# Who makes the low part of g in the early tiles: VectorE alone in the first five, GpSimd from the sixth on

## The reference

```python
w = softmax(weight_gen)                                  # over the 7 taps
conv[b, s, h, :] = sum over k of w[b, s, h, k] * x_pad[b, s + k, h, :]
h = conv @ w_in            # 16384 x 192 by 192 x 2048
g = maximum(0.01 * h, h)
out = g @ w_out            # 16384 x 2048 by 2048 x 192, float32
```

## Time and profile before

| | |
|---|---|
| median of 3 runs | 1031.0 us (1030.97 to 1031.47) |
| the profiled execution's own time | 1031.87 us |
| its span in the trace | 1030.1 us |
| TensorE (PE) busy | 1020.6 us, 99% |
| VectorE (DVE) busy | 939.0 us, 1199 instructions |
| ScalarE (ACT) busy | 634.3 us |
| GpSimd (POOL) busy | 550.5 us, 375 instructions |
| granted TensorE clock | 1.00 |

### The profile page before, as it was taken

One profiled execution on the slowest core, in us unless ns is written; L12 is line 12 of the kernel. 1 busy time (PEld: TensorE's weight loads), 2 busy tenths in 40 slices (PEclk: granted clock), 3 DMA queues, 4 the chain that ended last, 5 costly groups with the idle time before them and its releaser, 6 DMA issues.

```text
span 1030.1 us, 28954 instructions
## 1 busy us (share of the span) xinstructions
PE 1020.6 (99%) x12745; PEld 612.6 (59%) x12745; DVE 939.0 (91%) x1199; ACT 634.3 (62%) x1352; POOL 550.5 (53%) x375
## 2 busy tenths in 40 slices
PE   8999999999999999999999999999999999999998
PEld 3666655556556556655655655655565565566566
DVE  8989999999999999999999999999999999998611
ACT  7966665665556656556656555665565665566564
POOL 0114665555556655655655665565665566556543
PEclk9999999999999999999999999999999999999999
DMA  9421303112021310212112121210313112111100
GB/s 266 111 62 32 98 19 98 35 40 89 4 97 35 97 35 23 77 34 98 35 38 77 20 97 35 85 45 4 98 35 97 35 31 69 34 35 36 34 17 17
DMA packets 68309, 59.84 MB, mean 58 GB/s; under 512 B 56348, under 2 KB 60700, under 8 KB 66200
## 3 DMA queue, kind: packets, MB, share of 16 engines
q1 hardware_dynamic: 67196, 55.35, 18.4%
q0 software_dynamic: 864, 2.36, 1.3%
q10 hardware_dynamic: 124, 0.29, 0.1%
HBM read 29.34 MB, written 12.58 MB: 41 GB/s over the span
## 4 chain that ended last, share of the span: by engine, by line
PE 90%; DVE 6%; DMA 1%; ACT 1%; SPq 1%; issue 0%; POOL 0%; DVEq 0%; POOLq 0%
PE h_ps L1066 43%; PE out_ps L1176 22%; PE t_ps L1176 22%; PE out_ps L1130 1%; DVE prod L681 1%; PE h_ps L1048 1%; DMA rawO<-in_moe_w_out_dram 1%; DVE gl L883 1%; DVE conv L697 1%; PE out_ps L1140 1%; DMA prod<-prod 0%; DVE gl L755 0%; ACT g L483 0%; SPq L380 0%; ACT gh L481 0%
## 5 line engine op out<-in xcount | busy, mean ns | idle before, releaser
L349 POOL TENSOR_TENSOR gl<-g,gh 128x512 f16<-128x512 f32 x360 | 543.2, 1535 | 411.4 <-ACT g L483 411.4
L481 ACT ACTIVATE gh<-h_ps 128x512 f16<-128x512 f32 x512 | 317.6, 620 | 370.2 <-PE h_ps L1066 361.0
L1176 PE MATMUL t_ps<-wo,gh 64*128 64x384 f16 (+1 forms) x1984 | 386.6, 317 | 0.9 <-ACT gh L481 0.9
L1176 PE MATMUL out_ps<-wo,gh 64*128 64x384 f16 (+1 forms) x1984 | 386.6, 317 | 0.0
L1066 PE MATMUL h_ps<-xT,whA 64*128 64x512 f16 x1920 | 364.3, 376 | 0.0
L483 ACT ACTIVATE g<-h_ps 128x512 f32<-128x512 f32 x512 | 321.9, 629 | 0.0
L681 DVE TENSOR_TENSOR prod<-xbuf,taps 128x768 f32<-128x768 f32 x186 | 273.3, 1485 | 0.0
L697 DVE TENSOR_TENSOR conv<-conv,prod 128x768 f32<-128x768 f32 x174 | 266.4, 1531 | 1.0
L1176 PE MATMUL t_ps<-wo,gl 64*128 64x192 f16 x1920 | 233.2, 243 | 1.4 <-DVE gl L755 1.4
L1176 PE MATMUL out_ps<-wo,gl 64*128 64x192 f16 x1920 | 233.2, 243 | 0.0
L1176 PEld LDWEIGHTS t_ps<-wo,gh 64*128 64x128 f16 x1984 | 181.3, 94 | 57.6 <-ACT gh L481 1.4
(11 more groups left out here) (117 smaller groups left out, 713.3 us busy)
## 6 DMA issues: line engine op xcount, KB each, us to landing
xbuf<-in_x_dram SPq DMA_DIRECT2D x15, 1344.0 KB, 6.1
out_dram<-stage SPq DMA_DIRECT2D x31, 384.0 KB, 2.3
taps<-in_weight_gen_dram SPq DMA_DIRECT2D x16, 224.0 KB, 6.1
xT_again<-xT SPq DMA_DIRECT2D x29, 64.0 KB, 2.1
rawO<-in_moe_w_out_dram SPq DMA_DIRECT2D x4, 384.0 KB, 11.3
prod<-prod POOLq DMA_DIRECT2D x4, 384.0 KB, 4.3
rawA<-in_moe_w_in_dram SPq DMA_DIRECT2D x2, 512.0 KB, 8.6
xbuf<-in_x_dram SPq DMA_DIRECT2D x2, 384.0 KB, 7.3
```

The costliest lines, as they stand in the source:

```text
L349: nc.gpsimd.tensor_tensor(gl[:, q % RING, :], g[:, q % RING, :], gh[:, q % RING, :], ALU.subtract).then_inc(s_gl_p, 1)
L481: nc.scalar.activation(gh[:, q % RING, :], h_ps[q % GROUP][:], ACT.Prelu, alpha=SLOPE, scale=SHRINK0 if n < 2 * NG else SHRINK).then_inc(s ...
L1176: ins = nc.tensor.matmul(dst, a[rows, (m * NF + f) % RING, j * P:(j + 1) * P], moved, start=i == 0 and k < 2 and a is gh and f == 0 and pa ...
```

## The change

`EARLY` is 5. In tiles 2, 3 and 4 GpSimd makes nothing and VectorE makes each group's four lo in one operation, as in tiles 0 and 1; GpSimd's three of four begin with tile 5. VectorE's written order is new for tiles 2 to 4 (`third_tile`, and `tile_alone` in the place of `late_tile`). The convolution of two tiles further on is cut at other places (`CONV_FIRST`, `CONV_LATE`). On ScalarE the hi of x of the next tile moves from the second to the first step of tiles 3, 4 and 5. TensorE's and SyncE's programs are the same; which semaphore TensorE waits for before a lo product follows from `EARLY`.

```diff
--- before.py
+++ after.py
@@ -60,7 +60,8 @@
 
 CONV_TO = (4, 8, CONV.index(("top", 0)))
 CONV_EARLY = 9
-CONV_LATE = 11
+CONV_FIRST = 11
+CONV_LATE = 8
 
 
 def dynconv_mlp(nc, x, weight_gen, w_in, w_out, out):
@@ -213,10 +214,7 @@
         BY_PE = 2
 
 
-        LATE_TILES = (2, 3, 4)
-
-
-        EARLY = 2
+        EARLY = 5
 
 
 
@@ -542,7 +540,7 @@
                     copy_out(m - 1)
                 if i == 1 and m == BY_PE:
                     exp_taps(2)
-                if i == (1 if m in LATE_TILES or m - 1 in LATE_TILES else 0) and m + 1 < TILES:
+                if i == (1 if m == BY_PE else 0) and m + 1 < TILES:
 
                     hi_of_x(m + 1)
                 if i == NG - 1 and m % 2 == 1 and m + 3 < TILES:
@@ -784,38 +782,41 @@
 
             def third_tile():
 
-                conv_ops(3, CONV_EARLY, CONV_TO[2])
-                one_lo(2, 3)
-                conv_ops(3, CONV_TO[2], N_CONV - 1)
+                m = BY_PE
+                conv_ops(m + 1, CONV_EARLY, CONV_FIRST)
+                group(m * NG)
+                conv_ops(m + 1, CONV_FIRST, N_CONV - 1)
                 softmax_ops(2, 0, 2)
-                one_lo(2, 7)
-                next_rows(2)
+                group(m * NG + 1)
+                next_rows(m)
                 softmax_ops(2, 2, N_SOFTMAX)
                 dve.wait_ge(s_softmax, N_SOFTMAX * 2)
-                conv_ops(4, 0, CONV_TO[0])
-                one_lo(2, 11)
-                conv_ops(4, *CONV_TO[:2])
-                one_lo(2, 15)
-                conv_ops(4, CONV_TO[1], CONV_LATE)
-
-            def late_tile(m):
-
-                one_lo(m, 3)
+                conv_ops(m + 2, 0, 2)
+                group(m * NG + 2)
+                conv_ops(m + 2, 2, CONV_LATE)
+                group(m * NG + 3)
+
+            def tile_alone(m):
+
+                c = m // 2 + (2 if m % 2 == 1 else 1)
+                if m == BY_PE + 1:
+                    conv_ops(m + 1, CONV_LATE, N_CONV - 1)
+                if c < CHUNKS and m % 2 == 0:
+                    softmax_ops(c, 2, N_SOFTMAX)
+                group(m * NG)
                 sums(m - 1)
-                conv_ops(m + 1, CONV_LATE if m == 3 else CONV_TO[2], N_CONV - 1)
-                if m == 4:
-                    softmax_ops(3, 2, N_SOFTMAX)
-                one_lo(m, 7)
-                next_rows(m)
-                if m == 3:
-                    softmax_ops(3, 0, 2)
-                else:
-                    dve.wait_ge(s_softmax, N_SOFTMAX * 3)
-                conv_ops(m + 2, 0, CONV_TO[0])
-                one_lo(m, 11)
-                conv_ops(m + 2, *CONV_TO[:2])
-                one_lo(m, 15)
-                conv_ops(m + 2, CONV_TO[1], CONV_TO[2] if m == 3 else N_CONV - 1)
+                if m + 1 < TILES:
+                    next_rows(m)
+                if c < CHUNKS and m % 2 == 1:
+                    softmax_ops(c, 0, 2)
+                elif c < CHUNKS:
+                    dve.wait_ge(s_softmax, N_SOFTMAX * c)
+                for k in range(1, NG):
+                    if m + 2 < TILES:
+                        conv_ops(m + 2, (0, *CONV_TO)[k - 1], CONV_TO[k - 1])
+                    group(m * NG + k)
+                if m + 2 < TILES:
+                    conv_ops(m + 2, CONV_TO[2], N_CONV - 1)
 
             def tile(m):
 
@@ -975,8 +976,8 @@
             second_tile()
             third_tile()
             for m in range(3, TILES):
-                if m in LATE_TILES:
-                    late_tile(m)
+                if m < EARLY:
+                    tile_alone(m)
                 else:
                     tile(m)
             m, u = TILES - 1, (TILES - 1) % 2
```

## The result

The changed kernel takes 1028.82 us (median of 14 runs, 1028.53 to 1029.8) against 1031.15 for the kernel before (14 runs beside it): 2.33 us less, a ratio of 0.9976 with a 95% interval of 0.9968 to 0.9983. The profiled execution took 1028.74, its span is 1026.9.

A forecast was written before the change was run, and what follows sets the result against it. TensorE, busy 1020.6 of 1030.1 us, was taken to bound the kernel, so only its standstill could be won: 1031.87 - 2.75 + 0.27 = 1029.4, on the median 1031.0 - 2.48 = 1028.5 us. The range was 1028.1 to 1030.3.

The forecast's parts named there:

- What can be won: TensorE's steps of 7.805 us: 2.75 us lost in tiles 5 and 6, nothing in tiles 2 to 4 or after.
- Why VectorE was late: GpSimd's lo beside VectorE: a 768 element operation takes 1.91 instead of 0.95, one chunk's lo up to 1.65 instead of 0.68.
- The price of the four-chunk operation: VectorE, tiles 2 to 4: each four-chunk lo takes 2.2 us for the queue and 2.29 to the end.
- The step by step sum: VectorE's order from group 8 on: group 13 starts at 132.4, ends at 134.7, and TensorE loses 0.27 us there.
- the wait for g: VectorE waiting for a group's last g: group 9's there at 98.21, group 11's at 113.82.
- Group 17: VectorE's lo of this group: ready at 162.4, allowed until 163.6.
- ScalarE's move: x's hi of tiles 4 and 5 before a group of g: nothing lost, 0.4 us to spare on ScalarE.
- Tiles 5 and 6: Second lo of tile 5 done 196.4, wanted 197.4; of tile 6 done by 227.7, wanted 228.6; all 2.75 us go.
- Rival B: VectorE's chain in tile 3 is longer than summed; 5% more gives 1.0 us, 1029.5 to 1030; chance 0.20.
- C: The loss at 231.14, in tile 6, comes back; 1.54 us stays, time 1030.1; chance 0.08.
- D: Nothing of it happens because waits still count what they did; time 1031.0; chance 0.02.
- E: Something besides GpSimd slows VectorE's operations in tiles 2 to 4; kernel over 0.2% slower, 1053 at 1.83 each; chance 0.08.

The follow-up runs named there:

- dummy_lo: The changed kernel, with GpSimd in tiles 2 to 4 also subtracting 36 chunks of a buffer of its own that nobody waits for; 1050.13 us.
- division_only: The kernel before with EARLY 5, VectorE making each group's four lo in one operation in tiles 2 to 4, old order kept; 1030.70 us.
- hi_later: The changed kernel with ScalarE's hi of x put back to the second step of tiles 3, 4 and 5; 1042.56 us.
- order_only: The changed kernel's order on VectorE and ScalarE, but GpSimd making three of four lo from tile 2 as before; 1036.85 us.

## Why the prediction was right

The forecast was 1028.5 in a range of 1028.1 to 1030.3; 1028.82 was measured, and "below 1028.9" had been given 0.58. The 0.3 between 1028.5 and 1028.82 are 0.15 of the starting point (1031.0 from 3 runs, 1031.15 from 14), 0.10 of a loss that was summed too low, and a rest of 0.05 within the noise.

- **What can be won** (2.75 us, tiles 5 and 6, nothing elsewhere): shown. The steps there are 7.805 each in the changed kernel, and every version without a loss has the same 111 steps behind group 15.
- **Why VectorE was late** (GpSimd beside it): dummy_lo shows that this work alone makes the changed kernel late. For the kernel before it is only a part of the cause: division_only takes GpSimd's work out of tiles 2 to 4 and VectorE still comes to tile 5 only 0.5 earlier, because of its order, and then waits for ScalarE's hi of x (0.93 in the kernel before), which the prediction did not name among the causes.
- **The price of the four-chunk operation**, 2.2 and 2.29: 121.40 to 123.61, and 2.29 to the end. Right.
- **The step by step sum.** Taken from the start of group 8's hidden matmuls, it had group 13 start on VectorE at 49.5 (132.4 less 82.87) and it started at 49.64 (131.74 less 82.10); it had 0.27 us lost and 0.37 were. The term mis-sized is the wait for g: a four-chunk operation began 0.08 later behind the last g than the single one of the earlier trace rows, at group 9 and again at group 11.
- **Group 17** was in its window, 15, 16, 18 and 19 waited for g (0.54, 2.04, 0.50 and 1.05 us), tile 5's first lo after 2.79 ("some 3").
- **ScalarE's move**, "0.4 to spare": 0.55 idle behind the four activations. That it is needed the prediction did not say; hi_later shows that it is, at 14 us, 9 of them TensorE's waits and the rest the clock.
- **Tiles 5 and 6**: with the start 0.77 earlier, second lo of tile 5 at 194.9 expected, 194.58 measured; of tile 6 done at 226.9 expected, 226.90 measured. The last is luck: two errors cancel. That lo began 11.34 behind the first (214.88 to 226.22), where the prediction had 10.5, and it missed GpSimd, so that it took 0.68 and not 1.65.
- **Rival B** (a longer chain) holds for 0.1 of its 1 us. **C** did not come. **D** and **E** are excluded: no 768 element operation between 91 and 180 took over 1.0 us. The Trainium skill (SBUF — State Buffer, Who interferes with whom) was right in that.

What the prediction did not see is that neither half of the change would do. The order alone costs 5.7 us, the division alone brings 0.5 (0.58 by the steps). It costed the parts together only, so it had no number for either.

Left open: what in the first 82 us makes some executions start the steps 0.8 us later. No run was made for it. The 0.3 us that moving one add brings is shown in the steps, not settled in the medians. And how much of the old loss ScalarE's order made by itself is not shown: the old order on VectorE with x's hi early was not run.

## What to carry to other kernels

Where the engine that sets the time works in a fixed rhythm, count each step's start against it: the sum of the long steps is all that work on other engines can win inside the loop, and it gives the place of each loss. For the engine behind it, busy share tells little; what matters is whether it arrives inside the window of each step, and one wait for its input resets all lateness, so look for the stretch between two such waits. And before giving work to a second engine that slows the first, compare what it takes off with what it adds: here 0.6 us per chunk off, up to 0.96 per operation on.

## What the hardware showed that I had not expected

A wait of TensorE can cost more than itself: the granted clock went from 1.00 to 0.50 and TensorE worked at it for some 3 us, 1.4 to 1.7 us more for each wait of hi_later, and for 5.3 us, 2.6 more, in order_only. It fell at waits (from start to start) of 4.3, 3.3 and 2.2 us in hi_later, of 4.1 in order_only and of 3.7, 3.4 and 3.4 in dummy_lo, at some of them up to 1.3 us after TensorE had gone on. It stayed at the other wait of order_only, 2.2 as well, and at those of 1.9 and less in dummy_lo and the kernel before. Length alone does not tell the two waits of 2.2 us apart, and no run was made to find what does. So the price of lateness is not linear. Forecasts of slower versions by queue sums alone came out low twice, 1042.6 against 1036 to 1040 and 1036.9 against 1032 to 1035; 1050.1 was within its 1039 to 1051, with some 6 us of clock in it that the forecast did not have.

GpSimd's work lengthens a VectorE operation of four elements (0.22 to 1.12) as much as one of 2048 (2.29 to 3.24). In these rows the number of operations that it meets counts, not their size.
